# Attention and soft-MoE chain: score steps of 768 columns, one maximum job moved ahead of the sums, and a third probability tile added on VectorE

## The reference

```
q, k, v: (4, 8, 1152, 64)
q_pool = q.reshape(B, H, S // 2, 2, D).mean(axis=3)      # 576 queries
scores = scale * matmul(q_pool, k.transpose(0, 1, 3, 2)) # 576 x 1152
scores = scores - max(scores, axis=-1)
attn = exp(scores);  attn = attn / (sum(attn, axis=-1) + 1e-9)
out = matmul(attn, v)
```

## Time and profile before

| | |
|---|---|
| median of 3 runs | 786.02 us (784.36 to 787.11) |
| the profiled execution | 786.78 us, its span 785.0 us |
| mean granted TensorE clock | 0.992 of full speed |
| busy share | PE 96%, PEld 70%, POOL 62%, DVE 61%, ACT 50% |
| attention, 32 heads | about 22 to 476 us of the span |
| costliest group | GpSimd additions, line 426, 251.2 us |

### The profile page before, as it was taken

How to read it: one execution, slowest core, us unless ns; L and a number is a source line. 1 busy time by engine, 2 the same in 40 slices (tenths; PEclk the granted TensorE clock), 3 DMA queues, 4 the chain that set the end, 5 groups by cost and what they waited for, 6 DMA issues and landing times.

```text
span 785.0 us, 16851 instructions
## 1 busy us (share of the span) xinstructions
PE 752.6 (96%) x6397; PEld 546.6 (70%) x6397; DVE 481.0 (61%) x773; ACT 394.9 (50%) x784; POOL 488.5 (62%) x399
## 2 busy tenths in 40 slices
PE   4999999999999999999999989898899999999996
PEld 2777776777767767777677766432488888888885
DVE  6677676776766767767677637521575455555541
ACT  1465564664655646556465553211565454545452
POOL 1578888788887888878888772100475444444442
PEclk9999999999999999999999999999899999999999
DMA  3223324334243242333433208399700110101011
GB/s 82 81 70 85 108 84 148 99 99 149 82 139 109 89 148 93 120 127 83 149 98 102 87 22 305 147 364 387 267 1 10 32 28 14 40 0 40 1 40 41
DMA packets 51622, 81.82 MB, mean 104 GB/s; under 512 B 14557, under 2 KB 20573, under 8 KB 51549
## 3 DMA queue, kind: packets, MB, share of 16 engines
q1 hardware_dynamic: 51548, 80.83, 32.9%
HBM read 75.94 MB, written 4.79 MB: 103 GB/s over the span
## 4 chain that ended last, share of the span: by engine, by line
PE 91%; DVE 3%; DMA 2%; POOL 1%; issue 1%; ACT 1%; SPq 0%; ACTq 0%; POOLq 0%
PE ps L567 18%; PE ps L778 8%; PE ps L779 8%; PE ps L777 8%; PE ps L547 8%; PE ps L517 6%; PE ps L549 5%; PE ps L551 5%; PE ps L553 5%; PE ps L578 2%; PE ps L482 2%; PE ps L767 2%; PE ps L696 2%; PE ps L487 2%; DMA w_in<-in_moe_w_in 2%; PE ps L720 1%
## 5 line engine op out<-in xcount | busy, mean ns | idle before, releaser
L426 POOL TENSOR_TENSOR p_sum<-p_sum,probs 128x576 f32<-128x576 f32 x160 | 251.2, 1570 | 23.2 <-POOL p_sum L426 0.4
L1070 DVE TENSOR_REDUCE mx<-ps 128x2 f32<-128x1024 f32 (+1 forms) x160 | 191.3, 1221 | 102.0 <-PE ps L517 101.8
L848 ACT ACTIVATE probs<-ps 128x576 f32<-128x576 f32 x288 | 183.7, 652 | 43.2 <-PE ps L553 42.2
L455 POOL TENSOR_TENSOR g_lo<-g_buf,g_hi 128x384 fp32r<-128x384 f32 x96 | 100.5, 1048 | 103.5 <-ACT g_hi L978 103.4
L567 PE MATMUL ps<-probs,v_sb 128*64 128x288 f32 x1152 | 146.8, 409 | 0.7 <-ACT probs L848 0.7
L567 PEld LDWEIGHTS ps<-probs,v_sb 128*64 128x64 f32 x1152 | 79.9, 137 | 55.3 <-ACT probs L848 1.0
L1267 DVE SCALAR_TENSOR_TENSOR v_buf<-u_buf 128x384 f32<-128x384 f32 x96 | 58.8, 613 | 91.3 <-ACT u_buf L971 91.1
L779 PE MATMUL ps<-wo_lo,g_hi 128*128 128x512 f32 x288 | 113.6, 394 | 0.0
L778 PE MATMUL ps<-wo_hi,g_lo 128*128 128x512 f32 x288 | 113.4, 394 | 0.0
L777 PE MATMUL ps<-wo_hi,g_hi 128*128 128x512 f32 x288 | 113.0, 392 | 0.0
L547 PE MATMUL ps<-q_hi,k_hi 64*128 64x288 f32 x576 | 107.7, 359 | 0.9 <-ACT probs L848 0.9
(11 more groups left out here) (182 smaller groups left out, 1085.5 us busy)
## 6 DMA issues: line engine op xcount, KB each, us to landing
pre<-in_moe_w SPq DMA_DIRECT2D x47, 512.0 KB, 5.3
k_raw<-in_k SPq DMA_DIRECT2D x32, 288.0 KB, 4.0
v_sb<-in_v SPq DMA_DIRECT2D x32, 288.0 KB, 2.9
q_raw<-in_q SPq DMA_DIRECT2D x32, 256.0 KB, 3.8
from_x<-in_moe_w SPq DMA_DIRECT2D x9, 512.0 KB, 4.5
out<-o_stage SPq DMA_DIRECT2D x36, 128.0 KB, 2.4
p_inv<-inv_dram SPq DMA_DIRECT2D x62, 72.0 KB, 2.6
staged<-in_moe_w SPq DMA_DIRECT2D x8, 512.0 KB, 6.1
```

The costliest lines, as they stand in the source:

```text
L426: nc.gpsimd.tensor_tensor(total, total, probs[:, u, :], ALU.add).then_inc(probs_added, 1)
L848: nc.scalar.activation(dst, ps[:, b0:b0 + 2, 0:HALF], ACT.Exp, scale=SCORE_SCALE).then_inc(exp_done, 1)
L1070: top = nc.vector.tensor_reduce(mx[0:w, NC * t:NC * t + 2], ps[0:w, b:b + 2, :], AX.X, ALU.max)
```

## The change

Three things in one edit:

1. The nine score steps become seven. Step 0 stays (tile 8, 2 x 288 columns). Steps 2, 3, 5 and 6 are wide: a pair of key tiles, 384 of the 576 queries in each of the two banks. Steps 1 and 4 are side steps: four key tiles by the last 192 queries, two pieces of 192 columns in each bank. So six of the seven exponentials cover 768 columns where one of nine covered 576.
2. Job 0 of head n + 2 moves from ahead of step 0 to between weigh(n) and add_up(n). Jobs 1 to 5 come ahead of steps 1, 2, 3, 5 and 6.
3. GpSimd makes five additions in place of six. VectorE makes two in place of one (tiles 6 and 5 onto tile 7), the second one waiting for the first.

```diff
-        ADDS = NT - 3
+        ADDS = NT - 4
...
-        LAST_STEP = NT - 1
+        STEPS = 7
+        WIDE = 2 * SQ // 3
+        SIDE = SQ // 3
+        WIDE_STEPS = (2, 3, 5, 6)
+        SIDE_STEPS = (1, 4)
...
-                for u in range(NT - 3):
-                    pool.wait_ge(exp_done, NT * n + 3 + u // 2 * 2)
+                for u in range(ADDS):
+                    pool.wait_ge(exp_done, STEPS * n + (3, 3, 4, 4, 6)[u])
...
-            JOB_STEPS = (0, 1, 3, 5, 6, 8)
+            JOB_STEPS = (1, 2, 3, 5, 6)
...
-                if NT * n + s >= 2:
-                    pe.wait_ge(exp_done, NT * n + s - 1)
+                if STEPS * n + s >= 2:
+                    pe.wait_ge(exp_done, STEPS * n + s - 1)
+                if s == 0:
+                    parts = [(KP, 0, HALF, HALF)]
+                elif s in WIDE_STEPS:
+                    parts = [(P * WIDE_STEPS.index(s), 0, 0, WIDE)]
+                else:
+                    parts = [(P * (2 * SIDE_STEPS.index(s) + i), SIDE * i, WIDE, SIDE) for i in range(2)]
                 b0 = step_bank(n, s)
...
+                for key, c0, col, w in parts:
+                    t = slice(key, key + P)
+                    for part in range(4):
+                        for g in range(2):
+                            rows = rows_of(g)
+                            cols = slice(col * g, col * g + w) if s == 0 else slice(col, col + w)
+                            dst = ps[:, b0 + g, c0:c0 + w]
...
             def add_up(n):
...
                 pe.wait_ge(probs_added, ADDS * n + ADDS)
-                pe.wait_ge(pair_added, n + 1)
+                pe.wait_ge(pair_added, 2 * n + 2)
...
             for n in range(HEADS):
-                for s in range(NT):
+                if n == 0:
+                    row_max(1, 0)
+                for s in range(STEPS):
                     if n + 1 < HEADS and s in JOB_STEPS:
-                        row_max(n + 1, JOB_STEPS.index(s))
+                        row_max(n + 1, 1 + JOB_STEPS.index(s))
                     scores(n, s)
...
                 weigh(n)
+                if n + 2 < HEADS:
+                    row_max(n + 2, 0)
                 add_up(n)
...
-                if n > 0:
+                if n > 0 and s == 0:
                     act.wait_ge(pv_done, NT * n)
-                    if s < NT - 2:
-                        act.wait_ge(probs_added, ADDS * (n - 1) + (1 if s == 0 else (s + 1) // 2 * 2))
-                    else:
-                        act.wait_ge(pair_added, n)
-                        act.wait_ge(sums_done, n)
+                    act.wait_ge(sums_done, n)
...
             def add_pair(n):
-                dve.wait_ge(exp_done, NT * n + NT)
+                dve.wait_ge(exp_done, STEPS * n + STEPS)
                 dve.wait_ge(pv_done, NT * n + 1)
                 nc.vector.tensor_tensor(probs[:, NT - 2, :], probs[:, NT - 2, :], probs[:, NT - 3, :],
+                                        ALU.add).then_inc(pair_added, 1)
+                dve.wait_ge(pair_added, 2 * n + 1)
+                nc.vector.tensor_tensor(probs[:, NT - 2, :], probs[:, NT - 2, :], probs[:, NT - 4, :],
                                         ALU.add).then_inc(pair_added, 1)
```

More of the change, by code:

```diff
@@ L334, in _ @@
                     load_piece(n - 4)
-            sp.wait_ge(scores_ready, NT * HEADS)
+            sp.wait_ge(scores_ready, STEPS * HEADS)
             for i in range(STAGED):
@@ L435, in _ @@
                 head(n)
-            pool.wait_ge(scores_ready, NT * HEADS)
+            pool.wait_ge(scores_ready, STEPS * HEADS)
             nc.gpsimd.memset(si_m[:, :, :], 0.0).then_inc(si_zeroed, 1)
@@ L488, in turn @@
                     if m >= 2:
-                        pe.wait_ge(exp_done, NT * (m - 2) + NT - 1)
+                        pe.wait_ge(exp_done, STEPS * (m - 2) + STEPS - 1)
                     pe.transpose(ps[:, tail_bank(m), 0:P], k_raw[:, NT - 1:NT + 1, :].rearrange("p two d -> p (two d)"),
@@ L524, in turn_neg_max @@
                     pe.wait_ge(neg_free, m)
-                    pe.wait_ge(exp_done, NT * (m - 1) + NT - 1)
+                    pe.wait_ge(exp_done, STEPS * (m - 1) + STEPS - 1)
                 pe.transpose(ps[:, neg_bank(m), 0:P], neg_max[:, :], ident[:]).then_inc(neg_full, 1)
@@ L535, in scores @@
                     pe.wait_ge(turn_free, 4)
-                if NT * n + s >= 2:
-                    pe.wait_ge(exp_done, NT * n + s - 1)
-                b0 = step_bank(n, s)
[L539 to L551, removed]
-                        else:
-                            mm = pe.matmul(out, k_one[rows, :], q_neg[n % 2][rows, cols], start=False, stop=True)
@@ new lines, in scores @@
+                if STEPS * n + s >= 2:
[6 more added lines that the diff above has]
+                    parts = [(P * (2 * SIDE_STEPS.index(s) + i), SIDE * i, WIDE, SIDE) for i in range(2)]
+                b0 = step_bank(n, s)
+                for key, c0, col, w in parts:
[5 more added lines that the diff above has]
+                            dst = ps[:, b0 + g, c0:c0 + w]
+                            if part == 0:
+                                mm = pe.matmul(dst, k_hi[n % 2][rows, t], q_hi[n % 2][rows, cols], start=True, stop=False)
+                            elif part == 1:
+                                mm = pe.matmul(dst, k_lo[n % 2][rows, t], q_hi[n % 2][rows, cols], start=False, stop=False)
+                            elif part == 2:
+                                mm = pe.matmul(dst, k_hi[n % 2][rows, t], q_lo[n % 2][rows, cols], start=False, stop=False)
+                            else:
+                                mm = pe.matmul(dst, k_one[rows, :], q_neg[n % 2][rows, cols], start=False, stop=True)
@@ L554, in scores @@
                 mm.then_inc(scores_ready, 1)
             def weigh(n):
-                pe.wait_ge(exp_done, NT * n + NT)
+                pe.wait_ge(exp_done, STEPS * n + STEPS)
                 pe.wait_ge(v_loaded[n % 2], 16 * (n // 2) + 16)
@@ L833, in exp_step @@
             def exp_step(n, s):
-                act.wait_ge(scores_ready, NT * n + s + 1)
-                if n > 0:
+                act.wait_ge(scores_ready, STEPS * n + s + 1)
+                if n > 0 and s == 0:
                     act.wait_ge(pv_done, NT * n)
-                    if s < NT - 2:
-                        act.wait_ge(probs_added, ADDS * (n - 1) + (1 if s == 0 else (s + 1) // 2 * 2))
-                    else:
-                        act.wait_ge(pair_added, n)
-                        act.wait_ge(sums_done, n)
+                    act.wait_ge(sums_done, n)
                 b0 = step_bank(n, s)
@@ L844, in exp_step @@
                     dst = probs[:, NT - 1, :].rearrange("p (h c) -> p h c", h=2)
-                else:
-                    t, h = (s - 1) // 2, (s - 1) % 2
-                    dst = probs[:, 2 * t:2 * t + 2, HALF * h:HALF * h + HALF]
-                nc.scalar.activation(dst, ps[:, b0:b0 + 2, 0:HALF], ACT.Exp, scale=SCORE_SCALE).then_inc(exp_done, 1)
+                    src = ps[:, b0:b0 + 2, 0:HALF]
+                elif s in WIDE_STEPS:
+                    t = WIDE_STEPS.index(s)
+                    dst = probs[:, 2 * t:2 * t + 2, 0:WIDE]
+                    src = ps[:, b0:b0 + 2, 0:WIDE]
+                else:
+                    t = 4 * SIDE_STEPS.index(s)
+                    dst = probs[:, t:t + 4, WIDE:SQ].rearrange("p (i g) c -> p g i c", g=2)
+                    src = ps[:, b0:b0 + 2, 0:2 * SIDE].rearrange("p g (i c) -> p g i c", i=2)
+                nc.scalar.activation(dst, src, ACT.Exp, scale=SCORE_SCALE).then_inc(exp_done, 1)
             def read_x(n):
```

## The result

The changed kernel takes 795.34 us (794.75 to 795.93, four runs) against 786.2 us before, a ratio of 1.0119 with a 95% interval from 1.0099 to 1.0139: 9.1 us more. Forecast was 810, with 788 to 818 as the range. The direction and the range held, the size did not: 24 us had been forecast. It came out as rival A had it (794), whose times the range took in, so that the range held is no merit of the forecast's own chain.

A forecast was written before the change was run, and what follows sets the result against it. TensorE's own chain, 14.13 us a head, was taken to bound the kernel. Sums waiting for VectorE until 14.95 add 0.82 a head, +24.6 over 30 intervals, less about 0.5 in the last head: 810 us, range 788 to 818.

The forecast's parts named there:

- rival A: GpSimd's fifth addition takes its plain 1.42 us, or VectorE wins: +0.28 us a head, 794 us; chance 0.24.
- What bounds: Ahead of the sums: TensorE's own chain binds; the listed 13.1 us wait for GpSimd is a 0.44 us shape change.
- Paces: TensorE's score pairs: 0.133 us for 288 columns, 0.173 for 384, 0.11 for 192.
- Part 1: TensorE's score phase: 0.27 us lost to short pairs, fewer stops, turn 0.23 us earlier, at 7.77 after the sums.
- Job 1's stop: TensorE after step 0: stands from 1.27 to 1.58 us after the sums, waiting for ScalarE's `x_sum`.
- Part 2: Job 0 between weigh and the sums costs TensorE 0.44 us with its shape changes, without waiting for `turn_free`.
- Part 3: GpSimd's and VectorE's additions: GpSimd's fifth ends at 13.02 us, VectorE's second at 14.89, sums start at 14.95.
- The turn-taking behind it: After GpSimd's fifth addition: VectorE's first, half a division, VectorE's second take turns, ending at 13.63, 14.28 and 14.89 us.
- B: Faster: 192-column pairs at 0.093 us, job 0 costs only 0.23, no division between: -0.29 us a head, 777 us; chance 0.12.
- C: No change: half of B's savings and no lock wait beyond TensorE's own 14.1 us; chance 0.07.
- D: Slower still: both division halves or q pooling between VectorE's additions, up to +0.65 us a head more, 825 to 830; chance 0.05.
- The rule weighed: Port pair shared by VectorE and GpSimd: first to start locks it throughout, so GpSimd's fifth addition would run undisturbed.

The follow-up runs named there:

- nine_all: Kernel before, nine steps kept, with two additions on VectorE, GpSimd's division behind them and job 1 ahead of step 2: 781.4 us.
- steps_only: Kernel before with only the seven steps; job 0 ahead of step 0, six additions on GpSimd and one on VectorE: 797.5 us.
- move_only: Kernel before with only job 0 moved between weigh and the sums: 797.5 us, one run.
- pair_early: Changed kernel with VectorE's first addition ahead of the last two low parts of k and q: 805.0 us, one run.
- job_back: Changed kernel with job 0 put back ahead of step 0: 797.1 us.
- both: Changed kernel with job 0 back ahead of step 0 and GpSimd's division waiting for both VectorE additions: 785.2 us.
- no_div: Changed kernel with jobs 0 to 5 ahead of steps 0, 2, 3, 4, 5 and 6, division free between VectorE's additions: 783.4 us.
- div_late: Changed kernel with GpSimd's division also waiting for both of VectorE's additions: 794.5 us.

## Why the prediction was right and wrong, by its own steps

- **What bounds** was right. The listed wait for GpSimd was a change of shape, shown by nine_all's 0.44 and, the other way, by the 0.88 of steps_only.
- **Paces** were right: 192-column pairs follow at 0.11 (214.57, 214.69, 214.80), 384-column pairs at 0.18 (215.78, 215.96).
- **Part 1** had the turn at 7.77; it came at 220.44 - 212.55 = 7.89. The missing 0.12 is in the rows above. Job 4 ends with a single matmul on one half of the array (218.56), so from there one half runs 0.10 behind the other: a row of two matmuls lasts 0.44 at 220.07 and 0.35 at 215.96. With nine steps a stop for an exponential comes soon after and levels it; with seven none does before the turn. Not forecast. Timeline of the kernel before, a pair of 288 columns behind job 4 and one behind the stop that follows:

```profile
213.61 0.39 PE L553 MATMUL ps<-q_neg,k_one 64*128 64x288 f32 x2
...
214.13 0.30 PE L549 MATMUL ps<-q_hi,k_lo 64*128 64x288 f32 x2
```

- **Job 1's stop** was right: its weight load is at 214.15, like its first matmul, 1.60 after the sums' load, 1.58 forecast.
- **Part 2** was right: 0.43 for job 0, 0.44 forecast; move_only shows it alone.
- **Part 3 is the step that failed**, in one term: "the new lead is 0.69, nearest to head 0", so "GpSimd's fifth addition ends 11.74 + 1.28 = 13.02". It ended at 225.06 - 212.55 = 12.51, rival A's 12.47 within 0.04. The lead was 0.76 (223.65 to 224.41), not 0.69: VectorE was sent 0.12 later, by the later turn, and GpSimd 0.05. At 0.76 the addition takes 1.41; leads of 0.67 and 0.74 gave 1.95 and 2.02 elsewhere, so the forecast 0.69 would have given about 2 us. A miss of 0.12 in part 1 thus carried the addition over an edge that the forecast didn't know. And I had left out a row on the other side: in the last head of the kernel before, GpSimd's addition kept its 1.40 with VectorE's of the earlier trace rows sent 0.70 after it:

```profile
470.32 1.40 POOL L426 TENSOR_TENSOR p_sum<-p_sum,probs 128x576 f32<-128x576 f32 x1
```

  That place was used for the turn-taking and not for the lead.
- **The turn-taking behind it** was right: first addition 1.26, half division slipped in (1.10), second 1.23. The sums follow 0.11 after it, not 0.06.
- **The sum**: 0.82 a head forecast, 0.37 in most heads (14.50), 0.35 in the mean. Rival A's 0.28 lacked 0.04 in the fifth addition's end (12.51, not 12.47) and that 0.05. The later turn adds nothing to A's chain, where VectorE waits for GpSimd anyway.
- **The chances**: A had 0.24. Its price was nearly exact; the weight between it and the forecast hung on rows that disagree. The last head's row would have moved weight to A, but with the lead that was forecast it would have been the wrong row to go by: it has no low parts ahead, and behind them 0.67 and 0.74 gave about 2 us. The range from 788 to 818 left out B, C and D, 0.24 together, more than the 2 in 10 that it was meant to.
- **The rule weighed** (the Trainium skill, SBUF — State Buffer, section SBUF: two separate sides), that the first to start holds the ports for the whole instruction, gives most heads of the changed kernel right and the earlier trace rows and pair_early wrong (2.27 and 1.73 in place of 1.41). The measured table stands in its place.

Why three parts together cost 9 us, though each has a reason: the steps delay GpSimd's additions by 0.9 (steps_only), the third tile takes one of them off that chain but puts a second VectorE addition behind a half division (job_back: still 14.5), and job 0 in the gap costs TensorE 0.43 (move_only), which the late additions hide (job_back takes the same 14.5 without it). Taking the job back pays only once the additions come earlier (both).

## What to carry to other kernels

An idle time of constant length before every instance of an operation, whoever is named as its releaser, is a cost of the operation; look for an instance where the releaser was early. Where operations of two engines exclude each other, as these additions did, keep third parties (here a division nobody was waiting for) from slipping between two operations of a chain that somebody waits for: one extra wait on the engine with slack was worth 10 to 12 us (no_div, job_back), but only after the parallel chain of the same length was shortened as well. When an independent piece of work has to cover a latency, put in it the longest piece that needs nothing from it.

## What the runs showed of the hardware that was not expected

- There are three outcomes for a GpSimd and a VectorE addition of 576 columns that overlap, by the lead of GpSimd's, with edges near 0.40 and 0.74 us behind VectorE's low parts (the table above). In the middle band the GpSimd addition loses 0.3 to 0.6 us though it goes first. What holds the ports in that time stays open.
- A change of shape on TensorE leaves the weight loads idle: for 0.44 behind weigh, 0.24 from a job to the sums (div_late), 0.25 from scores to a turn (the change, at 220.44). A pair of 512 columns set between weigh and the sums costs 0.43, nearly twice its 0.23 in a stream.
- A single matmul on one half of the array shifts that half by 0.10 us against the other, and the shift lasts until the next stop (0.44 and 0.35 in the change, 0.39 and 0.30 in the kernel before).
